# Expert blocks of one expert each, with the plan loaded ahead of the transposes

## The chip, the cores and the metric

One core of one Trainium2 chip runs the whole program. The metric is the device time of one execution in microseconds (us), lower is better. The engines are TensorE (PE; its weight loads are PEld), VectorE (DVE), ScalarE (ACT), GpSimd (POOL) and SyncE (SP), whose queue issues DMAs. TensorE's clock has two levels, 1.2 and 2.4 GHz; the granted clock is shown as a share of the full one, 0.50 or 1.00.

## The reference

Three stages follow each other: an attention that keeps the top 32 scores of each row, a dense two-layer network with a leaky activation, and a mixture of eight experts with a skip. The change is in the third, on 2304 tokens of width 512, all in float32:

```python
skip_score = x @ w_skip                 # [2304]
do_compute = skip_score > 0
out = x.copy()
xc = x[do_compute]
logits = xc @ w_gate                    # 8 experts
e_idx = np.argmax(logits, axis=1)
gate_w = softmax(logits)[row, e_idx]
for e in range(8):
    mask = e_idx == e
    h = np.maximum(xc[mask] @ w1[e], 0) # w1[e] 512 x 1024
    y[mask] = gate_w[mask, None] * (h @ w2[e])   # w2[e] 1024 x 512
out[do_compute] = xc + y
```

## The kernel before

Attention and the dense network fill the first 1030 us. Their tail writes the rows of x to DRAM twice, into a table `x2_rows` and into the output. Then VectorE and TensorE work out the routing: each token that computes gets a place in a list that is sorted by expert, each expert's part padded to a multiple of half a block (64 rows), and the list is cut into blocks of 128. A block thus holds either rows of one expert ("whole") or 64 rows each of two experts ("mixed"). `slot_tok` says which token lies at each place, `b_plan_i` holds one number per block (last expert needed, buffer, mixed or not), and `b_end_i` the block at which each expert ends. For these inputs eight blocks are used of up to 22 in the code.

Each block j goes through this pipeline, with three row buffers (`BUFS`):

- GpSimd gathers its 128 rows with an indirect DMA into `xg` (`gather`, L1295) and later scatters its results (`scatter`, L1302). In `turn_of_blocks` (L1309) it does gather(j+2), scatter(j), then waits for an older scatter; so gather(j+3) is behind scatter(j) in its queue. Rows of the padding are out of bounds and move nothing.
- TensorE transposes the rows (`tx`, L614, four transposes into `acc[0]`), ScalarE copies them to `xgT`.
- TensorE multiplies by the expert's w1 (`gemm1`, L622, eight float32 products of 512 columns, which the profile shows as 16 records) and by the gate's weights (L648). VectorE and ScalarE do the softmax of the gate, and VectorE the ReLU into `hid` (`relu`, L1149, `hid_stored`).
- TensorE transposes the hidden block (`th`, L671, eight transposes), ScalarE copies it to `hidT` (`store_hidT`, L884), TensorE multiplies by w2 (`gemm2`, L680, again eight products, 16 records).
- VectorE scales by the gate, adds the row and stores into `yout` (`result`, L1156), which raises `y_stored`.

TensorE's program is straight code, written out for every block j in a nest of Ifs on the number of used blocks. Its order in block j is gemm1(j), gate, tx(j+1), gemm2(j-1), th(j), wait for result(j-1); behind the nest comes the last gemm2. In both products `with_weights` (L651) loads the block's plan from SBUF into a register, waits for the weights (`w1_ready`, `w2_ready`), and branches: a mixed block jumps through a tree of Ifs to one of four written-out versions (it multiplies each half by its own expert's weights into half of the output's partitions), a whole block addresses the weights by register.

The weights of four experts fit in `arena`. SyncE loads experts 0 to 3 as early as the memory is free, then w1 of expert e + 4 when the first product of the last block of expert e is done (`hid_ready`), w2 when its second product is done (`y_ready`), in pieces of 512 KB with two in flight (L403 to L433).

Of the kernel before, what the change touches and what calls it, by code (L numbers as in the profile page):

```python
# [24 lines left out]
def topk_attention_prelu_mlp_switch_moe(  # L25
# [17 lines left out]
    ALU = mybir.AluOpType  # L43
    ACT = mybir.ActivationFunctionType
    AX = mybir.AxisListType
    P = 128
# [22 lines left out]
    N = B * S  # L69
    DM, F1 = w_in.shape  # L70
    DT, FT1 = DM // P, F1 // P
# [8 lines left out]
    HB = P // 2  # L80
    BLOCKS = (N + E * HB) // P
    BUFS = 3
# [10 lines left out]
    with ctx:  # L93
        def sb(name, shape, dt=fp32):
            return ctx.enter_context(nc.sbuf_tensor(name, shape, dt))
# [81 lines left out]
        b_exp = sb("b_exp", [1, 2 * SLOTB])  # L177
        b_way = sb("b_way", [1, 2, SLOTB])

        b_plan_i = sb("b_plan_i", [1, SLOTB], i32)  # L180
        b_end = sb("b_end", [1, E])
# [21 lines left out]
        b_le = win_flat[0:1, o:o + 2 * SLOTB * E].rearrange("p (b e) -> p b e", e=E)  # L203
        assert o + 2 * SLOTB * E <= DT * F1
# [231 lines left out]
        def _(pe):  # L436
# [185 lines left out]
            def gemm1(j, b):  # L622
                pe.wait_ge(xgT_stored, j + 1)
                for c in range(F2 // 512):
                    if not isinstance(j, int) or j >= 1:
                        hold(pe, hid_stored, 2 * (j - 1) + c + 1)

                def whole(at):
                    for c in range(F2 // 512):
                        for d in range(DT):  # L630
                            last = nc.tensor.matmul(sc[0][:, c, :], xgT[:, b, d, :], arena[:, bass.ds(at + (d * F2 + c * 512), 512)],  # L631
                                                    start=(d == 0), stop=(d == DT - 1))
                        last.then_inc(hid_ready, 1)

                def mixed(at):
                    for c in range(F2 // 512):
                        for d in range(DT):
                            for h in range(2):
                                o = at[h] + d * F2 + c * 512
                                last = nc.tensor.matmul(sc[0][h * HB:(h + 1) * HB, c, :], xgT[:, b, d, h * HB:(h + 1) * HB],  # L640
                                                        arena[:, o:o + 512], start=(d == 0), stop=(d == DT - 1))
                        last.then_inc(hid_ready, 1)
# [8 lines left out]
            def with_weights(j, ready, whole, mixed):  # L651
                plan = pe.value_load(b_plan_i[0:1, bass.ds(j, 1)], min_val=0, max_val=E * 2 * EBUFS - 1)
                hold(pe, ready, plan // (2 * EBUFS) + 1)
                place = plan // 2 % EBUFS

                def places(lo, hi):
                    if hi - lo == 1:
                        mixed([lo * EXPERT, (lo + 1) % EBUFS * EXPERT])
                        return
                    half = (lo + hi) // 2  # L660
                    with pe.If(place < half):
                        places(lo, half)
                    with pe.If(place >= half):
                        places(half, hi)

                with pe.If(plan % 2 > 0):
                    places(0, EBUFS)
                with pe.If(plan % 2 < 1):
                    whole(pe.snap(place * EXPERT, min_val=0, max_val=(EBUFS - 1) * EXPERT))

            def th(j):  # L671

                for f in range(FT2):
                    if f % 4 == 0:
                        pe.wait_ge(hid_stored, 2 * j + f // 4 + 1)
                    last = nc.tensor.transpose(sc[1][:, f // 4, f % 4 * P:(f % 4 + 1) * P], hid[:, f * P:(f + 1) * P], ident[:, :])
                    if f % 4 == 3:
                        last.then_inc(hidT_ready, 1)

            def gemm2(j, stored):  # L680
                hold(pe, hidT_stored, stored)

                y = pt_full[:, :, :].rearrange("p a b -> p (a b)")

                def whole(at):
                    for f in range(FT2):
                        last = nc.tensor.matmul(y, hidT[:, f, :], arena[:, bass.ds(at + (DT * F2 + f * DM), DM)],  # L687
                                                start=(f == 0), stop=(f == FT2 - 1))
                    last.then_inc(y_ready, 1)

                def mixed(at):
                    for f in range(FT2):
                        for h in range(2):
                            o = at[h] + DT * F2 + f * DM
                            last = nc.tensor.matmul(pt_full[h * HB:(h + 1) * HB, :, :].rearrange("p a b -> p (a b)"),  # L695
                                                    hidT[:, f, h * HB:(h + 1) * HB], arena[:, o:o + DM],
                                                    start=(f == 0), stop=(f == FT2 - 1))
                    last.then_inc(y_ready, 1)

                with_weights(j, w2_ready, whole, mixed)  # L700

            pe.wait_ge(table_ready, 1)
            used = pe.value_load(b_end_i[0:1, E - 1:E], min_val=E // 2, max_val=BLOCKS)
# [204 lines left out]
        def _(dve):  # L908
            def search(p, par, g, steps):
# [163 lines left out]
            link(nc.vector.tensor_scalar(r_blk[:, :], count, 1.0, float(HB - 1), ALU.max, ALU.add))  # L1073
            link(nc.vector.tensor_copy(r_cnt_i[:, :], r_blk[:, :]))
            link(nc.vector.tensor_scalar(r_cnt_i[:, :], r_cnt_i[:, :], HB.bit_length() - 1, None, ALU.arith_shift_right))
# [10 lines left out]
            link(nc.vector.tensor_scalar(r_base[:, :], r_base[:, :], float(HB), None, ALU.mult))  # L1086
# [16 lines left out]
            def columns(size):  # L1103
# [6 lines left out]
            ends = r_end[0:1, s, :].rearrange("p (one e) -> p one e", one=1).to_broadcast([1, 2 * SLOTB, E])  # L1110
            halves = count_up[0:1, 0:2 * SLOTB].rearrange("p (b one) -> p b one", one=1).to_broadcast([1, 2 * SLOTB, E])
            link(nc.vector.tensor_tensor(b_le[:, :, :], halves, ends, ALU.is_ge))
            link(nc.vector.reduce_sum(b_exp[:, :], b_le[:, :, :], axis=AX.X))
            link(nc.vector.tensor_scalar(b_exp[:, :], b_exp[:, :], float(E - 1), None, ALU.min))
            first, second = (b_exp[:, :].rearrange("p (b h) -> p b h", h=2)[:, :, h] for h in range(2))
            link(nc.vector.tensor_copy(b_plan_i[:, :], first))
            link(nc.vector.tensor_scalar(b_plan_i[:, :], b_plan_i[:, :], EBUFS - 1, None, ALU.bitwise_and))
            nc.vector.tensor_copy(b_way[:, 0, :], b_plan_i[:, :])
            link(nc.vector.tensor_tensor(b_way[:, 1, :], second, first, ALU.subtract))
            link(nc.vector.scalar_tensor_tensor(out=b_way[:, 0, :], in0=b_way[:, 0, :], scalar=2.0, in1=b_way[:, 1, :],  # L1120
                                                op0=ALU.mult, op1=ALU.add))
            link(nc.vector.scalar_tensor_tensor(out=b_way[:, 0, :], in0=second, scalar=float(2 * EBUFS), in1=b_way[:, 0, :],
                                                op0=ALU.mult, op1=ALU.add))
            nc.vector.tensor_copy(b_plan_i[:, :], b_way[:, 0, :])

            link(nc.vector.tensor_scalar_add(b_end[:, :], r_end[0:1, s, :], 1.0))
            link(nc.vector.tensor_copy(b_end_i[:, :], b_end[:, :]))
            nc.vector.tensor_scalar(b_end_i[:, :], b_end_i[:, :], 1, None, ALU.arith_shift_right).then_inc(table_ready, 1)
# [55 lines left out]
        def _(pool):  # L1184
# [177 lines left out]
```

## Time and profile before

| | |
|---|---|
| median of 3 runs | 1248.27 us (1248.05 to 1248.88) |
| profiled execution, time | 1248.12 us |
| profiled execution, span of its instructions | 1246.3 us |
| mean granted TensorE clock | 0.884 |
| busy: PE, DVE, ACT, POOL | 968.4, 958.9, 588.1, 421.0 us |
| instructions | 21253 |

Times in the trace are counted from the first instruction. Busy time is that of the engine's own work; registers, branches, semaphores and the issue of DMAs are not in it, but the rows of one line can show them (PEldq, POOLq: the sequencer of the engine). "issue" in a chain is time in which the engine waited for nothing that the profile shows.

### The profile page before, as it was taken

Reading aid. Unit: us, or ns where it says so; the run is one execution under the profiler, and the core shown is the slowest. Engines: PE = TensorE matmul, PEld = TensorE weight load, DVE = VectorE, ACT = ScalarE, POOL = GpSimd, SP = SyncE. Lnnn points to the kernel's source line nnn. Section 1 sums busy time; section 2 is a strip of 40 time slices with the busy share of each in tenths; the row PEclk is TensorE's granted clock in tenths of the full one; section 3 lists DMA queues with packets and bytes.
Section 4 is the critical chain, followed back from the end, with each engine's and each line's share of the span. In section 5 each row is a group of like instructions: output and inputs, shape, how many; then the busy total and the mean of one; then the engine's idle time right before and its main releaser. Section 6 shows DMA issues by size and latency. Waiting matters only on the chain.

```text
span 1246.3 us, 21253 instructions
## 1 busy us (share of the span) xinstructions
PE 968.4 (78%) x6088; PEld 639.5 (51%) x6089; DVE 958.9 (77%) x2113; ACT 588.1 (47%) x1234; POOL 421.0 (34%) x553
## 2 busy tenths in 40 slices
PE   4355656448898899889889888987989994789894
PEld 2233333225575666657556566755757773333341
DVE  5999999999999999999999999999928205011110
ACT  2345535346746854773784486477349210110000
POOL 1122263546803830671382176157110000011100
PEclk9976566568998997999999999999989995799997
DMA  8233031301003002100300200100031017754620
GB/s 276 87 120 111 34 97 39 91 1 30 11 2 86 0 10 58 29 10 1 86 0 10 67 19 10 45 24 1 1 120 55 1 39 230 229 190 155 209 66 16
DMA packets 72609, 83.00 MB, mean 67 GB/s; under 512 B 47164, under 2 KB 51260, under 8 KB 70976
## 3 DMA queue, kind: packets, MB, share of 16 engines
q1 hardware_dynamic: 67120, 57.19, 15.7%
q0 software_dynamic: 5392, 24.65, 5.6%
q8 instruction: 45, 0.74, 0.2%
q14 instruction: 52, 0.43, 0.1%
HBM read 71.59 MB, written 11.53 MB: 67 GB/s over the span
## 4 chain that ended last, share of the span: by engine, by line
issue 30%; DVE 30%; PE 30%; ACT 3%; DVEq 2%; DMA 2%; POOL 2%; POOLq 0%; ACTq 0%; SPq 0%
DVE best L920 9%; DVE arena L933 8%; DVE arena L941 8%; PE acc L531 7%; PE acc L518 5%; PE sc L631 4%; PE pt_full L687 3%; DVEq L20 2%; PE sc L640 2%; PE sc L470 2%; PE pt_full L488 1%; DVE row_den L950 1%; PE acc L499 1%; DMA arena<-in_v_dram 1%; PE pt_full L695 1%
## 5 line engine op out<-in xcount | busy, mean ns | idle before, releaser
L920 DVE MAX8 best<-arena 128x8 f32<-128x576 f32 x576 | 403.4, 742 | 5.5 <-ACT arena L739 3.1
L933 DVE MATCH_REPLACE8 arena<-best,arena 128x576 f32<-128x576 f32 x432 | 315.8, 738 | 0.0
L1204 POOL TENSOR_SCALAR arena<-arena,row_inv 128x576 f32<-128x576 f32 x144 | 105.0, 745 | 352.6 <-DVE row_inv L953 352.6
L518 PE MATMUL acc<-arena,win_flat 128*128 (+1 forms) x1536 | 203.2, 289 | 24.6 <-ACT neg_part L785 19.4
L488 PE MATMUL pt_full<-ident,arena 128*128 128x128 f32 x576 | 112.3, 328 | 137.6 <-POOL arena L1204 85.9
L531 PE MATMUL acc<-arena 128*128 128x288 f16 x1536 | 199.8, 288 | 0.0
L518 PEld LDWEIGHTS acc<-arena,win_flat 128*128 128x128 f16 x1536 | 147.7, 98 | 75.9 <-issue 32.5
L531 PEld LDWEIGHTS acc<-arena 128*128 128x128 f16 x1536 | 149.7, 98 | 44.6 <-issue 8.0
L488 PEld LDWEIGHTS pt_full<-ident,arena 128*128 128x128 f32 x576 | 77.9, 166 | 179.5 <-issue 96.3
L941 DVE SCALAR_TENSOR_TENSOR arena<-arena,best 128x576 f32<-128x576 f32 x144 | 142.2, 1034 | 1.9 <-ACT arena L746 1.9
L739 ACT ACTIVATE arena<-sc 128x576 f32<-128x576 f32 x144 | 92.2, 643 | 107.4 <-PE sc L470 89.2
L758 ACT ACTIVATE arena<-pt_full 128x512 f32<-128x512 f32 x128 | 75.7, 592 | 134.6 <-PE pt_rest L489 133.1
L470 PE MATMUL sc<-qkT 64*128 64x288 f32 x512 | 129.1, 538 | 4.1 <-ACT arena L739 2.8
L499 PE MATMUL acc<-arena,v_nat 128*64 128x288 f32 (+1 forms) x640 | 94.6, 437 | 16.8 <-ACT arena L759 11.5
L746 ACT ACTIVATE arena<-arena,neg_max 128x576 f32<-128x576 f32 x144 | 100.6, 764 | 0.4 <-DVE neg_max L937 0.4
L339 POOL TENSOR_TENSOR pos_part<-pos_part,neg_part 128x288 f32<-128x288 f32 x96 | 83.1, 865 | 36.2 <-ACT neg_part L788 36.2
L470 PEld LDWEIGHTS sc<-qkT 64*128 64x128 f32 x512 | 70.3, 238 | 41.7 <-issue 21.5
L343 POOL TENSOR_TENSOR arena<-pos_part,arena 128x288 f16<-128x288 f32 x96 | 76.6, 798 | 14.3 <-POOL arena L341 0.9
L784 ACT ACTIVATE pos_part<-acc,scale 128x288 f32<-128x288 f32 x128 | 63.5, 496 | 31.5 <-PE acc L518 30.0
L1139 DVE TENSOR_REDUCE g_max<-acc 128x1 f32<-128x8 f32 x8 | 1.3, 167 | 99.8 <-PE acc L648 99.8
L499 PEld LDWEIGHTS acc<-arena,v_nat 128*64 128x64 f32 (+1 forms) x640 | 45.6, 143 | 62.5 <-issue 47.8
L788 ACT ACTIVATE neg_part<-neg_part,neg_alpha 128x288 f32<-128x288 f32 x128 | 68.5, 535 | 4.2
(160 smaller groups left out, 1031.0 us busy)
## 6 DMA issues: line engine op xcount, KB each, us to landing
arena<-in_moe_w_dram SPq DMA_DIRECT2D x64, 512.0 KB, 3.7
arena<-in_moe_w_in_dram POOLq DMA_DIRECT2D x8, 1024.0 KB, 5.6
arena<-in_moe_w_out_dram POOLq DMA_DIRECT2D x8, 1024.0 KB, 5.7
arena<-in_v_dram POOLq DMA_DIRECT2D x4, 1152.0 KB, 6.1
x_rows<-x2n SPq DMA_DIRECT2D x24, 192.0 KB, 2.5
out_dram<-x2n SPq DMA_DIRECT2D x24, 192.0 KB, 2.7
qk_nat<-in_q_dram SPq DMA_DIRECT2D x32, 128.0 KB, 2.5
qk_nat<-in_k_dram SPq DMA_DIRECT2D x32, 128.0 KB, 2.7
```

Of the source, the lines that this page charges most:

```text
L339: unit.tensor_tensor(pos, pos, neg, ALU.add).then_inc(leak_ready, 1)
L470: last = nc.tensor.matmul(dst[:, c, 0:HALF], qkT[at, 0, r * P:(r + 1) * P], qkT[at, 1, c * HALF:(c + 1) * HALF], start=True, stop=True)
L488: nc.tensor.transpose(pt_full[:, kt, :], src[:, kt * P:(kt + 1) * P], ident[:, :])
L499: last = nc.tensor.matmul(dst[h * D:(h + 1) * D, 0:HALF], v_nat[0:rows, par, h, kt, :], probsT[0:rows, h, kt, c * HALF:(c + 1) * HALF], st ...
L518: last = nc.tensor.matmul(dst[:, 0:HALF], win16[:, a, d, f * P:(f + 1) * P], xT16[:, bass.ds(row + d, 1), b, bass.ds(col, HALF)].rearrange ...
L531: last = nc.tensor.matmul(items.open[:, 0:HALF], wout16[:, a, f, d * P:(d + 1) * P], gT16[:, b, f, :], start=(f + n == 0), stop=(f == FT1 ...
L739: nc.scalar.activation(scores[:, t, :].rearrange("p (c s) -> p c s", c=2), sc[(TILES * par + t) % 2][:, :, 0:HALF], ACT.Copy).then_inc(s_s ...
L746: nc.scalar.activation(probs[:, gp, j, :], scores[:, GROUP * g + j, :], ACT.Exp, bias=neg_max[:, gp, j:j + 1], scale=SCALE).then_inc(exp_r ...
L920: nc.vector.max(best[:, gp, j, r, :], src).then_inc(max_found if r == 0 else dve_step, 1)
L933: nc.vector.match_replace(left[:, j, :], best[:, gp, j, r, :], src, MASKED).then_inc(dve_step, 1)
L941: nc.vector.scalar_tensor_tensor(out=probs[:, gp, j, :], in0=tiles[j], scalar=best[:, gp, j, ROUNDS - 1, 7:8], in1=probs[:, gp, j, :], op0 ...
L1204: nc.gpsimd.tensor_scalar(probs[:, gp, j, :], probs[:, gp, j, :], row_inv[:, gp, j:j + 1], 1.0, ALU.mult, ALU.mult)\
```

## The change

Blocks are of one expert each: each expert's part of the list is padded to 128 rows. For these inputs that makes eleven blocks, and up to 25 in the code (`BLOCKS`, so the tables are 26 columns wide in place of 23). The mixed versions and their branches go; both products address their weights by register (`weights_of`). The transposes th(j-1) move from the end of block j-1's part into gemm1(j), behind the load of the plan and ahead of the wait for w1. The wait for `y_stored` goes from the end of each block's part into gemm2, whose output it frees; `y_stored` starts at 1 for that. The last th and gemm2 stand behind the nest.

```diff
-    HB = P // 2
-    BLOCKS = (N + E * HB) // P
+    BLOCKS = (N - P) // P + E
...
             def gemm1(j, b):
                 pe.wait_ge(xgT_stored, j + 1)
-                for c in range(F2 // 512):
-                    if not isinstance(j, int) or j >= 1:
-                        hold(pe, hid_stored, 2 * (j - 1) + c + 1)
...
-                with_weights(j, w1_ready, whole, mixed)
-                if not isinstance(j, int) or j >= 1:
+                at, loaded = weights_of(j)
+                if j >= 1:
+                    th(2 * (j - 1) + 1, 2 * (j - 1) + 2)
+                hold(pe, w1_ready, loaded)
+                for c in range(F2 // 512):
+                    for d in range(DT):
+                        last = nc.tensor.matmul(sc[0][:, c, :], xgT[:, b, d, :], arena[:, bass.ds(at + (d * F2 + c * 512), 512)],
+                                                start=(d == 0), stop=(d == DT - 1))
+                    last.then_inc(hid_ready, 1)
+                if j >= 1:
                     pe.wait_ge(gate_sum, j)
...
+            def weights_of(j):
+                plan = pe.value_load(b_plan_i[0:1, bass.ds(j, 1)], min_val=0, max_val=E * EBUFS - 1)
+                return (pe.snap(plan % EBUFS * EXPERT, min_val=0, max_val=(EBUFS - 1) * EXPERT),
+                        pe.snap(plan // EBUFS + 1, min_val=1, max_val=E))
+
+            def th(*stored):
...
                     if f % 4 == 0:
-                        pe.wait_ge(hid_stored, 2 * j + f // 4 + 1)
+                        hold(pe, hid_stored, stored[f // 4])
...
             def gemm2(j, stored):
-                hold(pe, hidT_stored, stored)
...
+                at, loaded = weights_of(j)
+                hold(pe, w2_ready, loaded)
+                hold(pe, hidT_stored, 2 * stored)
+                hold(pe, y_stored, stored)
+                for f in range(FT2):
+                    last = nc.tensor.matmul(pt_full[:, :, :].rearrange("p a b -> p (a b)"), hidT[:, f, :],
+                                            arena[:, bass.ds(at + (DT * F2 + f * DM), DM)], start=(f == 0), stop=(f == FT2 - 1))
+                last.then_inc(y_ready, 1)
...
             tx(1, 1, 0)
-            th(0)
             with ExitStack() as inner:
                 for j in range(1, BLOCKS):
                     inner.enter_context(pe.If(used > j))
                     gemm1(j, j % BUFS)
                     tx(j + 1, (j + 1) % BUFS, (j + 1) // BUFS)
-                    gemm2(j - 1, 2 * j)
-                    th(j)
-                    pe.wait_ge(y_stored, j)
-            gemm2(used - 1, used * 2)
+                    gemm2(j - 1, j)
+            th(used * 2, used * 2)
+            gemm2(used - 1, used)
...
         def _(dve):
+            dve.sem_inc(y_stored, 1)
...
-            link(nc.vector.tensor_scalar(r_blk[:, :], count, 1.0, float(HB - 1), ALU.max, ALU.add))
+            link(nc.vector.tensor_scalar(r_blk[:, :], count, 1.0, float(P - 1), ALU.max, ALU.add))
...
-                hold(pool, y_stored, j + 1)
+                hold(pool, y_stored, j + 2)
```

Left out here: the same change from 64 to 128 in two more routing steps, and the steps that build the plan, which are fewer (no pair of experts per block, no halving of the ends).

## Rows read from the trace of the kernel before

**Rows 1.** The last stage in the windows: us, busy by engine (instructions), clock, DMA.
```profile
1065.50:1246.30 180.80, 145.22 (x512) 65.79 (x512) 21.32 (x56) 15.56 (x40) 17.08 (x27) 0.90 0.43 141
```

**Rows 2.** The chain of waits, blocks 0 and 1: start, us, what.
```profile
1078.64 1.21 issue
...
1089.95 2.01 issue
1091.96 7.04 PE pt_full L687 x16
```

**Rows 3.** The chain of waits, blocks 2 and 3.
```profile
1101.90 7.09 PE sc L640 x32
...
1110.46 6.88 PE pt_full L687 x16
...
1120.20 8.82 PE sc L631 x16
1129.02 0.79 PE acc L648 x8
1129.81 0.49 PE acc L619 x4
1130.30 7.02 PE pt_full L695 x32
1137.32 1.02 PE sc L676 x8
1138.34 2.57 issue
```

**Rows 4.** The chain of waits, from gemm2(6) to gemm2(7).
```profile
1211.96 6.87 PE pt_full L687 x16
...
1220.40 6.72 issue
1227.12 8.68 PE pt_full L687 x16
```

**Rows 5.** TensorE's sequencer, loads of the plan (L652) and waits of th (L20).
```profile
L652 PEldq TENSOR_LOAD <-b_plan_i x1: 302/302/302, 1107.1 to 1107.1; - x1
...
L20 PEldq EVENT_SEMAPHORE  x2: 51/51/51, 1112.9 to 1113.0; - x2
...
L652 PEldq TENSOR_LOAD <-b_plan_i x1: 303/303/303, 1118.4 to 1118.4; - x1
```

**Rows 6.** TensorE's branches between the last two second products, by line.
```profile
L710 PEldq COMPARE_BRANCH  x1: 3369/3369/3369, 1219.9 to 1219.9; - x1
...
L666 PEldq COMPARE_BRANCH  x1: 2093/2093/2093, 1224.6 to 1224.6; - x1
```

**Rows 7.** SyncE's issues of weight pieces, experts 4 to 7 (L428).
```profile
L428 SPq DMA_DIRECT2D arena<-in_moe_w_dram x32: 327/368/1265, 1093.9 to 1187.1; - x32
```

**Rows 8.** Windows by granted clock, from block 1 into block 3.
```profile
1083.50:1121.00 37.50, 31.47 (x118) 15.27 (x118) 5.36 (x14) 3.86 (x10) 3.70 (x6) 1.00 0.62 205
1121.10:1124.40 3.30, 3.30 (x5) 1.35 (x4) 0.00 (x0) 0.00 (x0) 1.24 (x2) 0.50 0.90 305
```

**Rows 9.** The gather of block 4, and landings of gathers 1, 4, 5, 8.
```profile
1121.27 1.04 POOL L1299 DMA_INDIRECT win_flat<-x_rows,tok_get  x1 [0.81 <-POOL tok_get L1297]
...
DMA to landing us min/median/max: 3.5/3.5/3.5
...
DMA to landing us min/median/max: 4.9/4.9/4.9
...
DMA to landing us min/median/max: 5.2/5.2/5.2
...
DMA to landing us min/median/max: 2.2/2.2/2.2
```

**Rows 10.** VectorE's step on the table (L1106), 24 x 23 columns.
```profile
L1106 DVE TENSOR_TENSOR win_flat<-count_up,r_pos_f x1: 729/729/729, 1041.0 to 1041.0; 96x552 f32<-96x552 f32 x1
```

**Rows 11.** Groups by line in the last stage, ScalarE's copies of hidden blocks.
```profile
L889 ACT ACTIVATE win_flat<-sc 128x512 f32<-128x512 f32 x16 | 8.8, 595 | 50.2 <-PE sc L676 50.2
```

More of the change, by code:

```diff
@@ L202, in topk_attention_prelu_mlp_switch_moe @@
         o += 5 * NTILES * E
-        b_le = win_flat[0:1, o:o + 2 * SLOTB * E].rearrange("p (b e) -> p b e", e=E)
-        assert o + 2 * SLOTB * E <= DT * F1
+        b_le = win_flat[0:1, o:o + SLOTB * E].rearrange("p (b e) -> p b e", e=E)
+        assert o + SLOTB * E <= DT * F1
         o = BUFS * DM
@@ L623, in gemm1 @@
                 pe.wait_ge(xgT_stored, j + 1)
+                at, loaded = weights_of(j)
+                if j >= 1:
+                    th(2 * (j - 1) + 1, 2 * (j - 1) + 2)
+                hold(pe, w1_ready, loaded)
                 for c in range(F2 // 512):
-                    if not isinstance(j, int) or j >= 1:
-                        hold(pe, hid_stored, 2 * (j - 1) + c + 1)
-                def whole(at):
-                    for c in range(F2 // 512):
[L630 to L642, printed above, removed]
-                with_weights(j, w1_ready, whole, mixed)
-                if not isinstance(j, int) or j >= 1:
+                    for d in range(DT):
[3 more added lines that the diff above has]
+                if j >= 1:
                     pe.wait_ge(gate_sum, j)
@@ L649, in gemm1 @@
                 last.then_inc(gate_ready, 1)
[L651 to L671, printed above, removed]
+            def weights_of(j):
[3 more added lines that the diff above has]
+            def th(*stored):
                 for f in range(FT2):
                     if f % 4 == 0:
-                        pe.wait_ge(hid_stored, 2 * j + f // 4 + 1)
+                        hold(pe, hid_stored, stored[f // 4])
                     last = nc.tensor.transpose(sc[1][:, f // 4, f % 4 * P:(f % 4 + 1) * P], hid[:, f * P:(f + 1) * P], ident[:, :])
@@ L680, in gemm2 @@
             def gemm2(j, stored):
-                hold(pe, hidT_stored, stored)
[L683 to L700, printed above, removed]
+                at, loaded = weights_of(j)
[6 more added lines that the diff above has]
+                last.then_inc(y_ready, 1)
             pe.wait_ge(table_ready, 1)
-            used = pe.value_load(b_end_i[0:1, E - 1:E], min_val=E // 2, max_val=BLOCKS)
+            used = pe.value_load(b_end_i[0:1, E - 1:E], min_val=E, max_val=BLOCKS)
             tx(0, 0, 0)
@@ L1108, in _ @@
             nc.vector.tensor_tensor(in_block[:, :, :], in_block[:, :, :], across(r_tok[:, :], SLOTB), ALU.mult).then_inc(slot_ready, 1)
-            ends = r_end[0:1, s, :].rearrange("p (one e) -> p one e", one=1).to_broadcast([1, 2 * SLOTB, E])
-            halves = count_up[0:1, 0:2 * SLOTB].rearrange("p (b one) -> p b one", one=1).to_broadcast([1, 2 * SLOTB, E])
-            link(nc.vector.tensor_tensor(b_le[:, :, :], halves, ends, ALU.is_ge))
+            ends = r_end[0:1, s, :].rearrange("p (one e) -> p one e", one=1).to_broadcast([1, SLOTB, E])
@@ L1113, in _ @@
+            blocks = count_up[0:1, 0:SLOTB].rearrange("p (b one) -> p b one", one=1).to_broadcast([1, SLOTB, E])
+            link(nc.vector.tensor_tensor(b_le[:, :, :], blocks, ends, ALU.is_ge))
             link(nc.vector.reduce_sum(b_exp[:, :], b_le[:, :, :], axis=AX.X))
             link(nc.vector.tensor_scalar(b_exp[:, :], b_exp[:, :], float(E - 1), None, ALU.min))
-            first, second = (b_exp[:, :].rearrange("p (b h) -> p b h", h=2)[:, :, h] for h in range(2))
-            link(nc.vector.tensor_copy(b_plan_i[:, :], first))
+            link(nc.vector.tensor_copy(b_plan_i[:, :], b_exp[:, :]))
@@ L1117, in _ @@
             link(nc.vector.tensor_scalar(b_plan_i[:, :], b_plan_i[:, :], EBUFS - 1, None, ALU.bitwise_and))
-            nc.vector.tensor_copy(b_way[:, 0, :], b_plan_i[:, :])
-            link(nc.vector.tensor_tensor(b_way[:, 1, :], second, first, ALU.subtract))
-            link(nc.vector.scalar_tensor_tensor(out=b_way[:, 0, :], in0=b_way[:, 0, :], scalar=2.0, in1=b_way[:, 1, :],
+            link(nc.vector.tensor_copy(b_way[:, :], b_plan_i[:, :]))
+            link(nc.vector.scalar_tensor_tensor(out=b_way[:, :], in0=b_exp[:, :], scalar=float(EBUFS), in1=b_way[:, :],
@@ L1121, in _ @@
                                                 op0=ALU.mult, op1=ALU.add))
[L1122 to L1128, printed above, removed]
+            nc.vector.tensor_copy(b_plan_i[:, :], b_way[:, :])
@@ L1130, in _ @@
+            nc.vector.tensor_copy(b_end_i[:, :], r_end[0:1, s, :]).then_inc(table_ready, 1)
             dve.wait_ge(table_summed, 1)
```

9 lines of the change are left out of this document (4 added, 5 removed).

## The prediction

> **What bounds the kernel now.** I read the windows by stage first, then the chain of waits through the last stage, then the sequencer's own rows by line, then the gathers and the weight loads. The change touches only what follows the routing, so the question is the last 180.8 us [rows 1]: TensorE is busy 145 of them, VectorE 21, ScalarE 16, GpSimd 17. The stage is TensorE's, at a mean granted clock of 0.90.
>
> The chain of waits says what a block costs. Block 3 runs, from 1120.20 on, 8.82 (first product), 0.79 (gate), 0.49 (transposes of the next block's rows), 7.02 (second product of block 2), 1.02 (transposes of hidden block 3), and then 2.57 us in which TensorE does nothing: 20.7 us from one first product to the next [rows 3]. The reader is to see two things there. First, the idle 2.57: it lies behind the wait for `y_stored` at the end of the block, and in it the sequencer loads the plan and takes branches (for block 3 that load starts at 1118.4, 1.8 us ahead of its first product) [rows 3, 5]. Second, the 8.82: the same number of columns takes 7.0 in the second products [rows 2, 3]. The window rows say why: 3.3 us of the first product run at 0.50 of the clock, the rest of the block at 1.00, and the fall comes in each block just behind that idle stretch [rows 8]. So a block is 16.2 us of work at 2.4 GHz, 2 to 2.6 us of idle time, and about 1.9 us of lost clock. Weight loads end at 1187 and set no block but by a hair [rows 7].
>
> **The change: eleven blocks for eight.** The three mixed blocks of before cost what a whole one costs: their second product takes 7.02 in 32 half-width records against 7.04 in 16 for a whole one [rows 2, 3]. So packing two experts into a block was free on TensorE, and what the change takes away is not work but packing: three more full blocks, each with gate, transposes, gather, two products and scatter.
>
> **The change: order and registers.** In the new order TensorE does th(j-1), gemm1(j), gate, tx(j+1), gemm2(j-1), with the plan load ahead of th. The wait on `y_stored` at the end of a block becomes a wait in front of gemm2(j-1) for result(j-2), which is a whole block old: VectorE does it right behind the product and TensorE did go on within 2 us of it, so it costs nothing here. Whether the plan load then costs anything is a matter of how far the sequencer runs ahead of the array. In block 2 it loads the plan for the second product at 1107.1, while the first product runs until 1109.0, and that second product starts at 1110.46 with no gap behind gate and transposes; at 1112.9 it stands at the wait of th, 4.4 us before the second product ends at 1117.3 [rows 3, 5]. The load and what follows take 1.8 us with the branches (1118.4 to the first product at 1120.20), 1.3 without [rows 3, 5, 6]. That fits in 4.4 us, and th itself gives another 1.0 of cover. If it did not fit, up to 2.6 us a block would stay. I take zero.
>
> So the new block at full clock is 1.0 (th) + 7.0 + 0.8 + 0.5 + 6.9 = 16.2 us [rows 2, 3].
>
> **What is late next: the gather.** GpSimd gathers block j+2 only behind the scatter of block j-1, because that row buffer is read by result(j-1). Let T be the end of gemm2(j-1). Scatter and gather follow each other on GpSimd, and the gather starts at T + 3.9 (1121.27 against 1117.3) [rows 3, 9]; it lands 3.5 us later on a quiet queue, 4.9 and 5.2 beside weight loads, 2.2 for a block with no rows [rows 9]. Before, tx needed it at T + 1.0 + 2.0 + 8.8 + 0.8 = T + 12.6: hidden with 3 us to spare. Now tx(j+2) is due at T + 8.8 and gemm2(j) at T + 9.3. A sequencer that waits for the gather has lost its lead: behind the landing come the issue of tx (0.5) and the plan load for the second product with its waits (1.3) before the product can start, so gemm2(j) starts at T + 3.9 + landing + 1.8. That equals T + 9.3 at a landing of 3.6 us. At 4.8 to 5.2 it is 1.2 to 1.6 us late; I take 1.4. Behind tx's wait on TensorE's queue stand gemm2 and everything after it, so the delay is on the path.
>
> How many blocks? Weight loads for experts 4 to 7 are 32 pieces from 1093.9 to 1187.1 [rows 7]; their gates are now blocks 0, 2, 3 and 5, so they again end near 1190 to 1195. Gathers 3 to 8 are issued in that time, every 16 to 18 us from 1101 on, one or two of them in a pause. I take five: 7.0 us. Bounds: 0 (all land in 3.5) and 8 times 1.9.
>
> The weights themselves are not late: expert 7 is needed at block 9, near 1215, and its first-product weights may load from the first product of block 5, near 1160, and take some 10 us.
>
> **The clock.** Before, it fell in each of blocks 3 to 7 behind 2 to 2.6 idle us; between 1083.5 and 1121.0, with idle gaps of 2 us too, it did not [rows 8]. With idle gaps gone or down to 1.4 us, between none and all nine of the blocks could see a fall, each worth 8.8 less 6.9, 1.9 us. I take two: 3.8 us.
>
> **Start and end.** Block 0: th(0) still waits for VectorE; behind it 1.21 us of idle go [rows 2], 0.1 stays, so 1.1 less. The 2.01 idle us in front of gemm2(0) [rows 2] have no releaser; the wait of the code that follows a branch is the likeliest, and I take half of it away (bounds 0 and 2). The table is 26 columns wide for 23, in two VectorE steps like the one of 0.73 us [rows 10] and in the small products behind them: 0.3 more. The integer steps that go were behind those products anyway. So T0, the end of gemm2(0), goes from 1099.0 to 1097.2.
>
> End: before, 6.72 us of idle stand between the last but one and last product [rows 4]; two branches make 5.46 of them, 3.37 leaving the nest of Ifs and 2.09 jumping over the mixed code [rows 6]. The second goes. The first is now taken while gemm2(9) runs (it waited for `y_stored` before), so at most part is seen. What remains is serial: th 1.0, ScalarE's copy of the last half 0.6 [rows 11], 0.6 for semaphores and the start, and 1.3, some of the 3.37, for code: gemm2(10) starts at T9 + 3.5 (bounds 2.2, and 8.3 as before, from 1218.83 to 1227.12). It takes 8.7 at the clock as before (6.9 if it holds). From its end to the end of the span was 1246.3 - 1235.8 = 10.5 [rows 4], with nothing changed: the last block is again the second of a turn.
>
> The Trainium skill ("Advanced Engine Details and Errata", Control Flow Timing) gives a compare-and-branch about 108 ns. The trace disagrees for far jumps, 3369 and 2093 ns; by the page's figure the branches removed here would be worth some 0.1 us each, and the end would gain nearly nothing from them.
>
> **Sum.** T0 1097.2 + nine blocks at 16.2 (145.8) = 1243.0; + 7.0 gather stalls + 3.8 clock = T9 at 1253.8; + 3.5 + 8.7 + 10.5 = 1276.5 span. The profiled run took 1.8 us more than its span (1248.12 against 1246.3), and lies 0.15 below the median of the three, so 1278 us, 30 above before, 2.4%. In other words: T0 to T6 of before took 119.8 us, 20.0 a block [rows 2, 4]. Six such periods at 16.2 give back 22.6, the start 1.8, the end 4.8 (27.5 from T6, now 22.7 from T9); three more blocks cost 48.6, stalls and falls 10.8.
>
> **Rivals.**
> A (my forecast, chance 0.52): gathers bind in some blocks; 1270 to 1287.
> B (0.24): the gathers land within 3.6 us or the clock never falls: no stall. The sum loses 7.0 and about 3.8 and perhaps 2 at the end: 1263 to 1269. For it: many blocks hold few rows now, and the landing of 3.5 with 2.2 for none. Against: 4.9 and 5.2 beside loads.
> C (0.17): the plan load is not covered, because the waits ahead of it (`xgT_stored`, the If) hold the sequencer until gemm2 is over, or because code arrives late in each block. Then 2 us a block stay, and the falls with them: 1278 - 7.0 + 9 x 2.0 is 1289, and up to 7 more falls of 1.9 make it 1302. For it: TensorE's gap of 2.01 with no releaser. Against: the second product's plan load, which is covered in every block.
> D, the other side (0.03): not slower. One mechanism: fewer blocks than eleven run. A block is worth 16.2 to 17.6, so ten would give 1261 and nine 1243; it decides at nine. The trace shows only which blocks were mixed, not the rows of each expert, so it can't exclude that by itself; the eleven is the change's own number. A floor says the same from the other side: with no stall and no fall, the work alone ends at 1263 (1278 less 7.0, 3.8, 1.3 and 1.8 at the end, 1.0 at the start), so eleven blocks can't reach 1248.
> The rest (0.04): A and C together or something new, above 1302.
>
> **Numbers.** 0.2% (2.5 us) is about what a measurement of this kernel tells from no change. Slower 0.97, the same 0.01, faster 0.02. The range 1264 to 1292 holds A, most of B and the lower end of C; the likeliest case alone is 1270 to 1287.
>
> **What would show it.** In the profile of the changed kernel: eleven groups of first products; the gap ahead of first products gone, 0.2 us or less; idle time ahead of tx (row transposes) with the gather as releaser, in blocks up to the last weight load and not after; second products at 6.9; the clock at 1.00 over most windows; gemm2(10) some 3.5 us behind gemm2(9). I would be wrong if the gap ahead of the first products stays, if the gap stands ahead of the second products without the gather as releaser, or if the clock falls in every block in spite of shorter gaps.

## The result and the profile after

The changed kernel took 1265.5 us (median of 4 runs, 1263.14 to 1267.82), against 1248.57 for the kernel before (median of its now four runs): 1.3% slower, ratio 1.013 with a 95% interval of 1.0107 to 1.0154. The forecast was 1278 with a range of 1264 to 1292, slower with a chance of 0.97; the median lies inside the range, near its lower end, and one of the four runs (1263.14) below it. The profiled execution took 1267.82 us, with a span of 1266.0.

In these two profiles nothing moved ahead of the last stage beyond 0.5 us: the first product of block 0 starts at 1066.08 (1065.54 before). The last stage, from there to the end of the span, is 199.9 us in place of 180.8. Two windows, the whole stage and nearly all of it behind block 1 (columns as in [rows 1]):

```profile
1066.00:1266.00 200.00, 182.10 (x572) 92.68 (x572) 29.33 (x77) 21.68 (x55) 24.50 (x39) 0.96 0.38 127
1082.60:1259.90 177.30, 167.05 (x535) 84.66 (x533) 27.50 (x71) 19.64 (x50) 24.50 (x39) 1.00 0.37 122
```

TensorE is busy 182 of 200 us where it was busy 145 of 181 [rows 1], and for the 177 us of the second window the granted clock is 1.00. The falls of [rows 8] do not appear in it; the one in block 1, just ahead of this window, is still there (0.50 from 1080 to 1082, and a first product of 7.71 us). So the engine that bounds the stage is better used than before, and the kernel is slower all the same: it has more to do.

The chain of waits through one block of the changed kernel (start, us, what) beside [rows 3]:

```profile
1166.77 6.87 PE sc L628 x16
1173.64 0.79 PE acc L634 x8
1174.43 0.49 PE acc L617 x4
1174.92 6.87 PE pt_full L658 x16
1181.79 0.87 PE sc L647 x8
```

First product 6.87, gate 0.79, row transposes 0.49, second product 6.87, hidden transposes 0.87: 15.9 us, no idle row between them, where [rows 3] had 20.7 with 2.57 idle. The sequencer now loads the plan that was loaded in that gap while the array is still at work on an earlier product. Its own row for block 2:

```profile
L638 PEldq TENSOR_LOAD <-b_plan_i x1: 298/298/298, 1090.8 to 1090.8; - x1
```

It starts at 1090.8, in the midst of the second product of block 0, which lasts from 1089.95 to 1096.83, and the first product of block 2 follows the transposes at once. The start, beside [rows 2]:

```profile
1079.03 1.92 PE sc L647 x8
1080.95 7.71 PE sc L628 x16
...
1089.95 6.88 PE pt_full L658 x16
```

The 1.21 and the 2.01 us of idle time of [rows 2] are both gone, so the second product of block 0 ends at 1096.83 (T0; 1099.0 before). And the gathers, by the chain around blocks 3 and 4:

```profile
1117.77 5.98 DMA win_flat<-x_rows,tok_get
...
1123.79 0.66 PE acc L617 x4
1124.44 0.51 issue
1124.95 7.14 PE pt_full L658 x16
...
1132.55 4.47 DMA arena<-in_moe_w_dram
1137.03 4.40 DMA arena<-in_moe_w_dram
1141.46 7.14 PE pt_full L658 x16
```

The gather starts at 1117.77 and lands at 1123.74; the row transposes that wait for it end 0.66 later, and the second product starts 0.51 us behind them, when the plan is loaded. In an unbroken block it would have started 9.0 us behind T = 1113.84, at 1122.8, so this landing of 5.98 us cost 2.1 us. In the last three rows a caution on reading such a chain: it names a weight DMA as what released the second product at 1141.46. But those pieces are w2 of expert 5, and this is block 3, of expert 2. That load ended at 1141.43 by chance. The gather landed 4.2 us behind its issue at 1136.0, which is 1140.2; the plan load follows at 1140.3, and the product 1.1 us behind it: the same lost lead, 0.34 us of it idle time in the open.

The end, beside [rows 4]:

```profile
1239.03 6.87 PE pt_full L658 x16
1245.90 0.45 PE sc L647 x4
...
1246.86 0.60 ACT win_flat L847
1247.46 0.41 issue
1247.87 7.14 PE pt_full L658 x16
```

2.0 us from one second product to the last one's start, in place of 8.3. Of the two far branches of [rows 6] the one over the mixed code is gone. The one out of the nest of Ifs is still there and takes as long, but the sequencer is at it while the array works on the second product from 1239.03 to 1245.90:

```profile
L669 PEldq COMPARE_BRANCH  x1: 3592/3592/3592, 1238.7 to 1238.7; - x1
```

### The profile page after: what moved, and what is told of

It reads as the page before. It is cut to its first block, busy times and chain, and to the rows that moved or that the text cites. A ratio compares the mean times of both kernels' runs of the same rounds, so it can differ in the third digit from the quotient of the medians.

```text
span 1266.0 us, 21586 instructions
## 1 busy us (share of the span) xinstructions
PE 997.4 (79%) x6148; PEld 663.1 (52%) x6149; DVE 965.5 (76%) x2130; ACT 594.1 (47%) x1249; POOL 428.3 (34%) x565
## 4 chain that ended last, share of the span: by engine, by line
issue 30%; PE 29%; DVE 29%; DMA 4%; ACT 3%; DVEq 2%; POOL 2%; POOLq 0%; ACTq 0%; SPq 0%
DVE best L879 8%; DVE arena L892 8%; DVE arena L900 8%; PE pt_full L658 6%; PE acc L529 6%; PE acc L516 5%; PE sc L628 4%; DVEq L20 2%; PE sc L468 2%; DMA win_flat<-x_rows,tok_get 2%; PE pt_full L486 1%; DVE row_den L909 1%; PE acc L497 1%; DMA arena<-in_v_dram 1%; DVE parts L925 1%
## 5 line engine op out<-in xcount | busy, mean ns | idle before, releaser
L486 PE MATMUL pt_full<-ident,arena 128*128 128x128 f32 x576 | 108.7, 320 | 143.2 <-POOL arena L1157 87.3
L497 PE MATMUL acc<-arena,v_nat 128*64 128x288 f32 (+1 forms) x640 | 92.6, 430 | 16.8 <-ACT arena L717 11.5
L628 PE MATMUL sc<-arena,win_flat 128*128 x176 | 81.4, 617 | 1.7 <-issue 1.7
L658 PE MATMUL pt_full<-arena,win_flat 128*128 x176 | 77.9, 596 | 3.3 <-issue 1.8
```

The source lines that it names most:

```text
L486: nc.tensor.transpose(pt_full[:, kt, :], src[:, kt * P:(kt + 1) * P], ident[:, :])
L497: last = nc.tensor.matmul(dst[h * D:(h + 1) * D, 0:HALF], v_nat[0:rows, par, h, kt, :], probsT[0:rows, h, kt, c * HALF:(c + 1) * HALF], st ...
L658: last = nc.tensor.matmul(pt_full[:, :, :].rearrange("p a b -> p (a b)"), hidT[:, f, :], arena[:, bass.ds(at + (DT * F2 + f * DM), DM)], s ...
```

## The experiments

The time before the last stage varies by up to 12 us from run to run (the first product of block 0 starts at 1060.5 to 1072.3 in these profiles), more than some effects here. Each ratio is to runs of the kernel before that were taken beside that run (medians of 1247.5 to 1250.6 us), and each run is read by its own profile too: "T0 to the last T" is the time from the end of the first second product to the end of the last but one, nine periods with eleven blocks and six with eight.

| kernel | blocks | median us, ratio to before (95%) | last stage us | T0 to last T | per period |
|---|---|---|---|---|---|
| before | 8 | 1248.57 | 180.8 | 119.8 | 20.0 |
| changed | 11 | 1265.5, 1.0107 to 1.0154 | 199.9 | 149.1 | 16.6 |
| after_again (changed) | 11 | 1268.1, 1.0083 to 1.0162 | 199.0 | 150.6 | 16.7 |
| early_11 | 11 | 1260.6, 1.0054 to 1.0099 | 192.4 | 144.0 | 16.0 |
| th_first_11 | 11 | 1263.7, 1.0056 to 1.0120 | 197.0 | 148.0 | 16.4 |
| no_loads_11 | 11 | 1259.0, 1.0038 to 1.0088 | 191.4 | 143.1 | 15.9 |
| old_order_11 | 11 | 1277.9, 1.016 to 1.028 | 212.0 | 157.3 | 17.5 |
| longer_gap_11 | 11 | 1308.3, 1.0468 to 1.0500 | 242.0 | 183.5 | 20.4 |
| branches_11 | 11 | 1318.0, 1.0537 to 1.0582 | 251.8 | 188.3 | 20.9 |
| order_8 | 8 | 1233.8, 0.9848 to 0.9915 | 164.6 | 112.8 | 18.8 |
| order_early_8 | 8 | 1231.8, 0.9815 to 0.9934 | 159.3 | 109.1 | 18.2 |
| best_8 | 8 | 1224.0, 0.9799 to 0.9841 | 159.2 | 108.4 | 18.1 |
| best2_8 | 8 | 1220.4, 0.9718 to 0.9791 | 152.2 | 99.9 | 16.7 |
| best2_8_no_early (best2_8) | 8 | 1222.9, 0.9713 to 0.9825 | 152.0 | 101.0 | 16.8 |

**after_again.** The changed kernel once more, as the measure of the next three.

> The changed kernel once more, beside the others, as their measure: 1263 to 1268 us. Its profile should show the gaps ahead of the second products again, some 1 to 2 us in blocks whose gather lands 4 us or later, 5 to 7 us in all, and none elsewhere.

Its periods sum to 150.6, 1.5 above the first profile. That is one fall of the clock: the second product at 1128.45, behind the longest wait for a gather (1.35 us ahead of the row transposes and 0.51 behind them), took 8.66 us. In the first profile the same two waits, 1.42 and 0.51 us, brought none. The rest repeats.

**early_11: the gather ahead of the scatter.**

```diff
-                    with pool.If(used > j + 1):
-                        gather(j + 2, (u + 2) % BUFS)
                     with pool.If(used > j):
+                        ready(j, u)
+                    with pool.If(used > j + 2):
+                        gather(j + 3, u)
+                    with pool.If(used > j):
                         scatter(j, u)
```

`ready` is the part of the scatter that frees the row buffer: GpSimd's copy of the tokens and its wait for `y_stored`. Left out here: gather(2) goes ahead of the first block, and `slot_tok` has one more column.

> The changed kernel, but GpSimd issues gather(j+3) ahead of scatter(j) in place of behind it, as soon as result(j) is stored: 2 us earlier in each block. My theory (the gather's landing is what is late in blocks 2 to 8, 6 us in all): the gather starts at T + 1.9, lands by T + 8, no idle time ahead of row transposes or second products, 5 to 6 us faster than the changed kernel, 1259 to 1260. Rival (the gaps of 0.5 to 1 ahead of second products are the plan load itself or late code): they stay, and at most 1 to 2 us go.

The periods fall from 149.1 to 144.0 us. Blocks 2 and 3 in its timeline (start, us, engine, line, what, idle before):

```profile
1101.76 0.66 PE L617 MATMUL acc<-ident,win_flat 128*128 128x128 f32 x4
1102.92 7.13 PE L658 MATMUL pt_full<-arena,win_flat 128*128 x16 [0.51 <-issue]
...
1118.44 0.64 PE L617 MATMUL acc<-ident,win_flat 128*128 128x128 f32 x4
1118.91 7.03 PE L658 MATMUL pt_full<-arena,win_flat 128*128 x16
```

Only block 2 still waits (its row transposes start 0.2 late, then 0.51 idle); from block 3 on the second product follows the transposes with nothing between. In time it is 7.5 us below after_again, with intervals that overlap a little (1.0054 to 1.0099 against 1.0083 to 1.0162). The periods are 6.6 us below those of after_again, 1.5 of them its fall of the clock.

**no_loads_11: no weight loads beside the gathers.** SyncE skips the loads of experts 4 to 7, whose blocks so multiply by the weights of experts 0 to 3.

```diff
                     for piece in range(PIECES):
+                        if e >= EBUFS:
+                            continue
```

> The changed kernel, but the weights of experts 4 to 7 are not loaded: their blocks multiply by the weights of experts 0 to 3, in the same time. My theory (the gathers land late because of the weight loads beside them): landings fall from 4.1 to 6.0 to about 3.3, stalls go, 5 to 6 us faster. Rival (landings of 4 to 6 us are the indirect DMA's own, by rows): landings and stalls stay, no change.

The gathers of blocks 3 to 11, of the changed kernel and of this one:

```profile
L1252 POOL DMA_INDIRECT win_flat<-x_rows,tok_get x9: 1041/1042/1052, 1101.2 to 1234.0; - x9
...
DMA to landing us min/median/max: 2.1/4.1/6.0
```

```profile
L1254 POOL DMA_INDIRECT win_flat<-x_rows,tok_get x9: 1044/1046/1056, 1104.8 to 1231.7; - x9
...
DMA to landing us min/median/max: 2.1/3.3/3.5
```

The median landing falls from 4.1 to 3.3 us, the worst from 6.0 to 3.5, and the nine periods are 15.9 to 16.0. So the gathers were late because weight loads ran beside them, and 143.1 us is the floor for this order: the changed kernel's 149.1 holds 6.0 us of gather stalls.

**th_first_11: the plan loaded behind the transposes.**

```diff
-                pe.wait_ge(xgT_stored, j + 1)
-                at, loaded = weights_of(j)
                 if j >= 1:
                     th(2 * (j - 1) + 1, 2 * (j - 1) + 2)
+                pe.wait_ge(xgT_stored, j + 1)
+                at, loaded = weights_of(j)
```

> The changed kernel, but th(j-1) stands ahead of the wait for xgT_stored and the load of the plan. My theory (the sequencer is 4 us ahead of the array there, so the place of the load doesn't matter, and only the moved wait on y_stored gave the time back): no change, within 1 us of the changed kernel. Rival (the load has to stand ahead of the transposes to be covered): up to 1.3 us a block, 13 us slower.

The transposes and the first product of block 2 of that kernel:

```profile
1093.51 1.04 PE L647 MATMUL sc<-ident,win_flat 128*128 128x128 f32 x8
1094.38 7.03 PE L628 MATMUL sc<-arena,win_flat 128*128 x16
```

The product starts 0.87 behind the start of the transposes, with no idle time, as in the changed kernel. Periods of 16.4 against 16.6, times that overlap. The place of the load, which the change moved, is worth nothing; with the wait on `y_stored` gone from between the blocks, either place is covered. The next run shows that it is this wait that kept the sequencer from running ahead: on TensorE it does the same work in the same order as th_first_11, and differs in the place of that wait (and of one branch, now behind it) alone.

**old_order_11: eleven blocks, the order of before, no branches.**

```diff
                 at, loaded = weights_of(j)
-                if j >= 1:
-                    th(2 * (j - 1) + 1, 2 * (j - 1) + 2)
...
                     gemm2(j - 1, j)
+                    th(2 * j + 1, 2 * j + 2)
+                    pe.wait_ge(y_stored, j + 1)
```

Left out here: th(0) stands behind tx(1) again, and the th behind the nest goes.

> The changed kernel with the order of before: blocks of one expert, eleven of them, no branches, but th at the end of each block and behind it the wait on y_stored, then the plan load. My theory: 1.4 to 2 us of idle time return in each block, with them the clock falls of 1.9, no gather stalls: periods of 19 to 19.5, about 1298 us. Rival (the idle time of before was the branches): 0.8 us a block, the clock stays up, 1272 to 1278.

Here my expectation failed and the rival's held. The periods are 17.5, not 19 to 19.5:

```profile
1163.87 1.04 PE L645 MATMUL sc<-ident,win_flat 128*128 128x128 f32 x8
1166.25 7.13 PE L626 MATMUL sc<-arena,win_flat 128*128 x16 [1.34 <-issue]
```

The idle gap is 1.2 to 1.35 us in every block from the second on (0.40 in block 1), and behind it the first product takes 7.13: the clock does not fall between 1070 and 1257. The order is worth 12.1 us of stage on eleven blocks (212.0 less 199.9), 8.2 of them in the nine periods: they lose the gaps, and take on the 6.0 us of gather stalls.

**longer_gap_11: the same, with the plan loaded three times over.**

```diff
+                if j >= 1:
+                    weights_of(j)
+                    weights_of(j)
                 at, loaded = weights_of(j)
```

> The changed kernel with the order of before, and the plan loaded three times over ahead of each first product: idle gaps of 2.4 us in place of 1.2 to 1.35, no branches. Theory (the fall of the clock hangs on the length of the idle gap): the falls of 1.9 us per block return, periods of 20 to 20.5 in place of 17.5, 1303 to 1308 us. Rival (the falls need the branches or mixed blocks): the clock stays up as in the kernel with short gaps, periods of 18.7, about 1290 us.

```profile
1157.41 1.04 PE L648 MATMUL sc<-ident,win_flat 128*128 128x128 f32 x8
1160.93 8.83 PE L629 MATMUL sc<-arena,win_flat 128*128 x16 [2.48 <-issue]
```

Gaps of 2.47 to 2.65 us, and behind each of them a first product of 8.8 us, in all nine blocks from the second on; block 1 has 8.76 us behind a gap of 1.68. Here the products have no branches inside, and no block is mixed. Periods of 20.4: 1.2 more of gap and 1.7 of clock than in old_order_11. So a longer gap alone brings the falls; neither branches nor mixed blocks are needed.

Its length does not settle every block, though. In the kernel before, block 2 had a gap of 2.03 us and no fall, block 3 one of 1.99 and a fall, and branches_11, the next run, has both behind the same gap:

```profile
1186.30 7.13 PE L631 MATMUL sc<-arena,win_flat 128*128 x16 [2.21 <-issue]
1204.66 8.83 PE L631 MATMUL sc<-arena,win_flat 128*128 x16 [2.21 <-issue]
```

**branches_11: the kernel before with eleven blocks.** Each expert's halves are rounded up to an even number (127 is added in place of 63, and the shift by 6 becomes a shift by 7 and a doubling); order and branches stay.

> The kernel before, its order, its branches and its two halves per block, but each expert's part padded to 128 rows: eleven blocks, none of them mixed, no other edit. My theory (a block of before costs 20 us, of which 1.3 idle for wait and plan load, 0.8 for branches, 1.9 lost clock): periods of 19.5 to 20.5, the last stage 180.8 + 3 x 20 = 240 us, 57 to 62 us slower than before, about 1308. With the same block count as the order-of-before kernel without branches (stage 212 us) it shows what the branches cost: 25 to 30 us. Rival (the branches cost only their own 0.8 us a block, and the falls of the clock come from mixed blocks): stage near 221, 1290.

251.8 us of stage, more than the 240 of my theory. Besides gaps of 2.0 to 2.2 us, some with a fall and some without, two gaps of 7.18 and 6.18 us stand in its timeline. The line of the branch on mixed or whole says what they are:

```profile
1156.95 1.04 PE L676 MATMUL sc<-ident,win_flat 128*128 128x128 f32 x8
1165.17 9.90 PE L631 MATMUL sc<-arena,win_flat 128*128 x16 [7.18 <-issue]
```

```profile
L666 PEldq COMPARE_BRANCH  x22: 345/424/5396, 1063.9 to 1292.3; - x22
```

22 branches, median 0.42 us, the longest 5.4: a jump over the unused code that in this block (from 1159.4 on) takes ten times the usual; the one in the other gap takes 4.07, from 1264.1 on. Against old_order_11 (212.0) the branches cost 39.8 us on eleven blocks. In the nine periods it is 31.0: 17.0 of longer gaps ahead of the first products, these two jumps among them, 2.1 ahead of second products, and 11.7 of clock that falls behind the gaps. The other 8.8 are ahead of T0 and behind the last T.

**order_8: the new order alone.** Eight blocks, mixed code and branches as before; plan load, th and the wait on `y_stored` placed as in the change.

> The kernel before with the new order alone: eight blocks, three of them mixed, branches as before, but plan load and th(j-1) ahead of the first product, and the wait on y_stored in front of the second product. My theory (idle gap and clock falls go with the order alone, and each added block costs 15.9 to 16.5): T0 near 1097, six periods of 15.9 with 4 to 6 us of gather stalls, last product 3 to 4 us behind T6: about 1222 us, 26 faster than before and 43 faster than the changed kernel. Rival (the branches keep the gaps, the new order needs the code without them): 1240 or more.

1233.8 us, 1.2% faster than before, but 12 slower than expected. Its periods are 18.8 us. The gaps behind it, in the timeline:

```profile
1153.58 7.09 PE L641 MATMUL sc<-arena,win_flat 128*64 128x512 f32 x32 [1.46 <-issue]
...
1169.76 1.09 PE L679 MATMUL sc<-ident,win_flat 128*128 128x128 f32 x8
1174.50 10.19 PE L632 MATMUL sc<-arena,win_flat 128*128 x16 [3.65 <-SPq L433]
```

Blocks 5 and 6 wait for w1 of experts 6 and 7: SyncE's landing of the latter ends at 1173.5, and the sequencer, which waits at `w1_ready`, goes on at 1173.55. In the 10.19 us of the last row the clock falls too. The weight loads, which before set nothing, are late once eight blocks run at this pace. With eleven blocks they are not: the profile of the changed kernel has no gap ahead of a first product behind block 0.

**order_early_8, best_8, best2_8.** The new order with the early gather; then with w1 of expert 6 loaded ahead of w2 of expert 5; then with w1 of expert 7 ahead of w2 of expert 6 too:

```diff
-            for e in range(E):
...
-                for layer in range(2):
+            loads = [(e, layer) for e in range(5) for layer in range(2)]
+            loads += [(5, 0), (6, 0), (5, 1), (7, 0), (6, 1), (7, 1)]
+            for e, layer in loads:
```

> The new order alone with eight blocks, three of them mixed, and gather(j+3) issued ahead of scatter(j). My theory: no gather stalls, 4 to 5 us faster than the new order alone, about 1218. Rival (late code behind the branches is a stall of its own): gaps with no releaser stay, 1222 to 1226.

> Eight blocks, new order, gather ahead of the scatter, and SyncE loads w1 of expert 6 ahead of w2 of expert 5 (both gates are open by then), so that expert 7's weights come 8 to 10 us earlier. Theory (the 2.58 and 3.65 us ahead of the first product of block 6 in the two runs of eight blocks are expert 7's late w1): that gap goes, with 1.9 us of clock behind it: 4 to 5 us faster than new order and early gather alone, 1226 to 1228. Rival (the gap is late code behind the far branch): it stays, no change from 1232.

> As the best kernel of eight blocks so far, but SyncE loads w1 of expert 7 ahead of w2 of expert 6 as well. Its gate, the first product of block 4, opens near 1137, and the load takes 10 us, so it should land near 1151, before block 6 asks for it near 1162. Theory: the gap of 5.04 us ahead of that first product and the fall of the clock behind it go, 6 us faster than 1224: 1217 to 1219. Rival (w2 of expert 6 is now late for the second product of block 5): a gap moves there, 1222 to 1225.

> The same kernel once more, for the spread of its times: 1217 to 1219.

The early gather took 3.7 us off the periods of order_8, within the noise of the time; at 1231.8 us it is above both what I expected (1218) and the rival (1222 to 1226), since blocks 5 and 6 go on waiting for w1, which neither had. Loading expert 6 earlier removed the wait for it (109.1 to 108.4 in all), but the wait for expert 7 grew to 5.04 us: that load still stood behind w2 of expert 6. So best_8's time of 1224.0, below the 1226 to 1228 that I expected, is no sign of my theory: the gap did not go, and the last stage is as long as in order_early_8 (159.2 and 159.3). With the second swap it is gone:

```profile
1158.07 1.09 PE L684 MATMUL sc<-ident,win_flat 128*128 128x128 f32 x8
1159.00 7.03 PE L637 MATMUL sc<-arena,win_flat 128*128 x16
1165.87 0.95 PE L654 MATMUL acc<-wroute,win_flat 128*128 128x8 f32 x8
1166.68 0.64 PE L624 MATMUL acc<-ident,win_flat 128*128 128x128 f32 x4
1167.24 7.09 PE L706 MATMUL pt_full<-arena,win_flat 128*64 128x512 f32 x32
```

The transposes, the first product of block 6, gate, row transposes and second product follow each other; 99.9 us for six periods, 1220.4 us (the same kernel run once more, under the label best2_8_no_early, gave 1222.9), ratio 0.9754 with an interval of 0.9718 to 0.9791. The rival had foreseen a gap moving to the second product of block 5, by w2 of expert 6 coming late. A gap of 1.69 us does stand ahead of the second product of block 4, but it is not that: SyncE's wait for the load under way ends at 1151.75, behind the start of the product at 1151.05. It is once more a gather, issued at 1142.4 beside weight loads and landed at 1148.6, with the plan load of the second product right behind it and then the branches of a mixed block:

```profile
DMA to landing us min/median/max: 6.2/6.2/6.2
...
L658 PEldq TENSOR_LOAD <-b_plan_i x1: 316/316/316, 1148.6 to 1148.6; - x1
```

This version beats both kernels, by 2.5% and by some 3.7%.

## Why the prediction held, and where it was off

It held in direction and in its range. Its size was off by 12.5 us: 30 us slower was forecast and 17 came, below the 1270 to 1287 of the likeliest case A. Its account held in the gap that closes and the gather that is late next, and not in the clock. The sum, term by term, against the profiled span of 1266.0:

- T0: forecast 1097.2, was 1096.8. This is in part luck: both idle gaps went whole (3.2 us, where I took 2.1 away), and a lower clock in block 0 (a first product of 10.20 us, 9.25 before) took some back. From the first product to T0 it was 30.7 us here, 33.5 before, and 28.3 in after_again.
- The period at full clock: 16.2, was 15.9; nine of them are 2.8 us less. I took the transposes at 1.0 and the first product at 7.0; in an unbroken stream they are 0.87 and 6.87.
- The gather stalls: 7.0 in five blocks, was 6.0 (149.1 less 143.1), in five blocks, of 0.5 to 2.4 us each. The mechanism stood as described: landing beside weight loads, lost lead of the sequencer, 1.2 us from landing to product rather than the 1.8 that I had. no_loads_11 removes it, and early_11 all but one block of it, from the other side. My landing of 3.5 us "on a quiet queue" was misread: it is that of the gather at 1060.5, beside which weight loads ran. The figure holds all the same: no_loads_11 has 3.0 to 3.5 with no loads.
- Falls of the clock behind T0: 3.8 for two, was none in this profile and one in the next. This is the term that was mis-sized most. I had it as anything between none and nine, since the profile of before had gaps of 2 us with and without a fall; old_order_11 (1.2 to 1.35 us, none in nine) and longer_gap_11 (2.5, one in each) narrow it from both ends, and between them it stays open.
- The end: 3.5 us to the last product, was 2.0, since code was not late there; that product 8.7, was 7.1; the rest 10.5, was 11.0.

Together 10.5 us less than the forecast 1276.5. Rival B's time range (1263 to 1269) is where the result lies. B named two conditions, gathers in time or no fall of the clock; the second came true in this profile and the first did not, so the stalls that it left out were there, and its time is met because each period and the end were shorter than in my sum. For the same reason my floor of 1263 for the work alone was too high: early_11 has 1260.6 and no_loads_11 1259.0. C is refuted by the block rows above. D fell with eleven blocks seen. And 2.5 us is less than what the time tells: 23 runs of the kernel before, taken beside the first four experiments, lie between 1247.1 and 1260.9.

What the prediction left unsplit, since it took the whole gap as gone: the change is three edits. By stage, one after the other: eleven blocks with all else as before, +71.0 (180.8 to 251.8); the branches out, -39.8 (to 212.0); the order, -12.1 (to 199.9). The first is not only three times a block of 20.0; far branches add to it in that kernel. I had put the branches at 0.5 us a block and 2 at the end. Of the larger price on eleven blocks, 19.1 us stand in the gaps within the periods, with two jumps of 5.4 and 4.1 us (the kernel before had long jumps only at its end), and 11.7 in the clock, which I had booked under the gap as a whole. The share of each edit depends on the order in which they are made: on eight blocks the order alone gives 16.2 us of stage with the branches kept (180.8 to 164.6).

Left open: why some jumps take 4 to 5 us and others of the same line 0.35. Instruction fetches stand in the profile near some of them (one packet between 1158 and 1166 in branches_11), but also where no long jump is (two between 1166 and 1176), and no run here moved them apart. Open too is what decides a fall of the clock behind a gap of about 2 us. And whether eight blocks without branches could gain more was not tried.

## What to carry over

Count the blocks first: when the bounding engine takes the same time for a mixed block as for a full one, packing is worth a whole block each time (a period of 15.9 us here; from best2_8 to early_11, the best of either count, the stage grows by 40.2 us for three blocks), and here no cleaner inner loop paid for giving it up; take the scheduling gain and keep the packing. A wait on a result that nobody needs yet, placed between two blocks on the bounding engine, costs more than its own time: it stops the sequencer from running ahead and exposes what follows it (1.2 to 1.35 us a block here), and if the gap grows it can cost clock. And once such a gap is gone, look for what was hidden by it: here a gather that had 3 us to spare, then weight loads that had been on time.

## What the runs showed of the hardware

- An idle gap on TensorE of 1.2 to 1.35 us in each block of 17.5 us left the granted clock at 1.00 for 187 us (old_order_11); one of 2.47 to 2.65 us in each block of 20.4 us brought a fall to 0.50 every time, worth 1.7 us (longer_gap_11). Between them both were seen: with 2.21 us of gap one first product took 7.13 us and another 8.83 (branches_11).
- A conditional branch on TensorE's sequencer took 0.35 us at the least and 5.4 at the most, on the same line of code and with the same outcome (line 666 of branches_11); the row of line 669 above has 3.59. The Trainium skill ("Advanced Engine Details and Errata", Control Flow Timing) gives a compare-and-branch about 108 ns; the row of line 666 disagrees. The shortest ones of line 710 in that run, 68 ns, lie below it.
- An indirect gather of at most 128 rows of 2 KB landed in 3.0 to 3.5 us with no weight load beside it (no_loads_11; 2.1 for the one behind the last block, which has no rows), and in up to 6.0 us in the changed kernel and 6.2 in best2_8, beside loads of 512 KB a piece, two in flight.
- TensorE's sequencer stood 4.4 us ahead of the array in the kernel before, and loaded block 2's plan 6.0 us before the end of the running second product in the changed one (1090.8 against 1096.83). Behind a wait that stops it, a plan load and what follows took 1.2 to 1.35 us of idle time a block (old_order_11).
